# Middle stage of a long-convolution kernel: block stores issued by ScalarE, two steps after a block's last turn, instead of by the sync engine

## The reference

```python
h_mlp = np.maximum(pos_emb @ w1, 0.0) @ w2
h_filt = h_mlp * np.exp(-0.01 * pos)[:, None]
u = x * v
L = 2 * S
y = irfft(rfft(u, n=L, axis=1) * rfft(h_filt, n=L, axis=0)[None], n=L, axis=1)[:, :S, :]
t = (x * y).reshape(B * S, D)
h = t @ w_in                                    # 128 -> 2048
P = a[0] + a[1] * h + a[2] * h**2 + a[3] * h**3
Q = 1.0 + abs(b[0]) * abs(h) + abs(b[1]) * h**2
out = (P / (Q + 1e-6)) @ w_out                  # 2048 -> 128
```

## Time and profile before

| | |
|---|---|
| median of 3 runs | 2010.45 us (2007.9 to 2017.58) |
| the profiled execution, its time | 2015.76 us |
| its span, first to last instruction | 2014.0 us |
| mean granted TensorE clock, share of full | 0.99 |
| PE busy | 1909.8 us (95%) |
| DVE busy | 1735.1 us (86%) |
| ACT busy | 1643.8 us (82%) |
| POOL busy | 1737.2 us (86%) |
| queue q1 (SP), share of 16 DMA engines over the span | 28.0% |
| queue q10 (ScalarE), likewise | 4.7% |

### The profile page before, as it was taken

The page is one execution under the profiler, slowest core; times in us unless marked ns, Lnnn a source line. Parts: engine busy times, 40 slices in busy tenths (PEclk is TensorE's granted clock), DMA queues, the critical chain, the costliest instruction groups (busy, mean ns, idle before and its releaser), DMA issues. The chain is left out here.

```text
span 2014.0 us, 27071 instructions
## 1 busy us (share of the span) xinstructions
PE 1909.8 (95%) x7898; PEld 1301.4 (65%) x7898; DVE 1735.1 (86%) x2375; ACT 1643.8 (82%) x2424; POOL 1737.2 (86%) x1226
## 2 busy tenths in 40 slices
PE   6998799999799999999999999999999999999997
PEld 4555467777566666666666666666666666666664
DVE  4555479999599999999999999999999999999997
ACT  1222246555499999999999999999999999999998
POOL 5555367777499999999999999999999999999997
PEclk9999999999999999999999999999999999999999
DMA  7888889999601111111111111111111111111100
GB/s 195 276 289 290 248 204 248 248 255 247 183 5 33 33 34 34 38 46 38 38 33 33 34 33 34 33 34 33 34 33 34 33 34 33 34 33 37 34 9 13
DMA packets 77517, 181.83 MB, mean 90 GB/s; under 512 B 15565, under 2 KB 19557, under 8 KB 74485
## 3 DMA queue, kind: packets, MB, share of 16 engines
q1 hardware_dynamic: 70717, 144.74, 28.0%
q10 hardware_dynamic: 6656, 35.39, 4.7%
HBM read 108.36 MB, written 71.76 MB: 89 GB/s over the span
## 5 line engine op out<-in xcount | busy, mean ns | idle before, releaser
L726 POOL TENSOR_TENSOR den<-slope,mag 128x832 f32<-128x832 f32 x480 | 947.4, 1974 | 0.0
L962 PE MATMUL acc_p<-g_s,w_out_k 128*128 128x416 f32 x1920 | 768.8, 523 | 43.1 <-DVE g_s L879 22.6
L846 DVE SCALAR_TENSOR_TENSOR num<-square,level,h_p 128x832 f32<-128x832 f32 x480 | 517.8, 1079 | 83.9 <-ACT square L757 41.7
L718 POOL TENSOR_SCALAR slope<-mag,den_c 128x832 f32<-128x832 f32 x480 | 500.2, 1042 | 60.1 <-DVE mag L841 43.0
L962 PEld LDWEIGHTS acc_p<-g_s,w_out_k 128*128 128x128 f32 x1920 | 342.1, 189 | 290.2 <-issue 183.9
L879 DVE SCALAR_TENSOR_TENSOR g_s<-num,ratio,r_p 128x832 f32<-128x832 f32 x480 | 518.0, 1079 | 11.6 <-ACT r_p L773 4.6
L757 ACT ACTIVATE square<-h_p,centre 128x832 f32<-128x832 f32 x480 | 469.0, 977 | 39.3 <-DVE mag L841 36.7
L951 PE MATMUL h_p<-xy_hi,w_lo 128*128 128x416 f32 x960 | 454.3, 473 | 7.0 <-DVE num L846 5.6
L766 ACT ACTIVATE den<-den 128x832 f32<-128x832 f32 x480 | 440.9, 919 | 1.7 <-POOL den L726 1.5
L773 ACT ACTIVATE r_p<-den 128x832 f32<-128x832 f32 x480 | 426.8, 889 | 0.9 <-DVE g_s L879 0.7
L951 PE MATMUL h_p<-xy_hi,w_hi 128*128 128x416 f32 x960 | 336.9, 351 | 0.0
(11 more groups left out here) (79 smaller groups left out, 2190.4 us busy)
## 6 DMA issues: line engine op xcount, KB each, us to landing
bin_s<-bent SPq DMA_DIRECT2D x23, 1440.0 KB, 10.8
bent<-bent_s ACTq DMA_DIRECT2D x28, 1152.0 KB, 9.8
x_s<-in_x SPq DMA_DIRECT2D x59, 416.0 KB
vin_s<-back SPq DMA_DIRECT2D x29, 768.0 KB, 5.9
back<-back_s SPq DMA_DIRECT2D x23, 960.0 KB, 12.8
v_s<-in_v SPq DMA_DIRECT2D x30, 416.0 KB
out<-o_s SPq DMA_DIRECT2D x60, 208.0 KB
merged_s<-table_merged SPq DMA_DIRECT2D x24, 225.0 KB, 4.1
```

Of the source, the lines that this page charges most:

```text
L718: nc.gpsimd.tensor_scalar(slope[:, q % DEEP], mag[:, q % DEEP], den_c[:, 1:2], den_c[:, 0:1], ALU.mult, ALU.add).then_inc(slope_done, 1)
L726: nc.gpsimd.tensor_tensor(den[:, q % DEEP], slope[:, q % DEEP], mag[:, q % DEEP], ALU.mult).then_inc(den_done, 1)
L846: nc.vector.scalar_tensor_tensor(out=num[:, q % NUMS], in0=square[:, q % SQUARES], scalar=level[:], in1=h_p[:, q % 2, :, 0:TOK], op0=ALU.a ...
L962: mm = nc.tensor.matmul(acc_p[:, 0:TOK], w_out_k[:, ft], g_s[:, q % DEEP, t], start=(ft == 0), stop=(ft == FT - 1))
```

## The change

`store` of the middle stage is taken out of SP's stream and put into ScalarE's. ScalarE issues the store of block b in its iteration k = 4(b+1) + 1, behind cos_part(k), that is two steps after the block's last turn. What it waits for, what it writes and the semaphore it counts are the same. The four stores of the last block and the wait for all stores at the end stay with SP.

```diff
--- before.py
+++ after.py
@@ -452,12 +452,6 @@
                     sp.dma_start(bin_s[:, s].rearrange("p k c f -> p k (c f)"),
                                  bent[blk * JB:(blk + 1) * JB].rearrange("k j f -> j k f")).then_inc(bin_in[s], 16)
 
-                def store(blk):
-                    s = blk % SLOTS
-                    sp.wait_ge(vturned, (blk + 1) * JB)
-                    sp.dma_start(back[:, blk * JB:(blk + 1) * JB, :],
-                                 back_s[:, s].rearrange("p k c f -> p k (c f)")).then_inc(back_out[s], 16)
-
                 load_merged(0)
                 for m in range(JB):
                     sp.dma_start(bin_s[:, 0, m].rearrange("p c f -> p (c f)"), bent[m]).then_inc(first_in[m], 16)
@@ -476,7 +470,6 @@
                                          (unfold_s, tab["unfold"]), (w_in_s, w_in),
                                          (w_out_s, w_out.rearrange("(t p) d -> p t d", p=128))):
                             sp.dma_start(dst[:], src).then_inc(later_in, 16)
-                    store(blk)
                 for m in range(JB):
                     k = (K_BLOCKS - 1) * JB + m
                     sp.wait_ge(vturned, k + 1)
@@ -523,6 +516,12 @@
                     act.wait_ge(v_done, k + 1)
                     nc.scalar.activation(vpart[:, k % 2], v_p[0:J, k % 2], ACT.Copy,
                                          scale=turn_j[:, k, 0:1]).then_inc(vpart_done, 1)
+
+                def store(blk):
+                    s = blk % SLOTS
+                    act.wait_ge(vturned, (blk + 1) * JB)
+                    nc.scalar.dma_start(back[:, blk * JB:(blk + 1) * JB, :],
+                                 back_s[:, s].rearrange("p k c f -> p k (c f)")).then_inc(back_out[s], 16)
 
                 act.wait_ge(spread_in, SPREAD)
                 nc.scalar.activation(spread_hi[:], spread_s[:], ACT.Copy).then_inc(split_done, 1)
@@ -533,6 +532,8 @@
                         split_y(k + LEAD_Y)
                     if inside(k):
                         cos_part(k)
+                    if k >= JB + 1 and k % JB == 1:
+                        store(k // JB - 1)
                 act.wait_ge(later_in, LATER)
                 nc.scalar.activation(w_hi[:], w_in_s[:], ACT.Copy).then_inc(split_done, 1)
```

## The result

The changed kernel takes 2025.03 us (median of 7 runs, 2017.82 to 2028.51) against 2010.45 before (7 runs, 2005.77 to 2017.58): the ratio, estimated over all runs (that of the two medians is 1.0073), is 1.0068, 95% interval 1.0049 to 1.0087. Run again beside the experiments it was 1.0048 (1.0030 to 1.0066). So it is slower, by 0.5 to 0.7%, 10 to 14 us. The forecast was +4 us.

What follows compares the result with a forecast made beforehand. The middle stage was taken as bound by TensorE, with DMA just below its limit. From 2015.8 us profiled, +5 for loads, -1 for TensorE's waits and 0 otherwise gave +4, so 2014.5 against the 2010.45 median; range 2005 to 2028.

Steps and rivals of the forecast that it cites:

- the rival priced from +10 on: Middle stage slower by over 0.5%: two queues at once make DMA less efficient; +10 to +24 us, chance 0.22.
- part 3, the load of bin_s: Store packets delay the load's tail past its 11.61 us deadline: 0.25 us a block, 21 loads, +5 us.
- The picture of every block a little late: Expected sign: load landings about 12 us, short TensorE waits every fourth step, SP's issues 10.9 to 11.0 us apart.
- What bounds the kernel, and the worth of the hidden waits: Middle stage: TensorE sets 10.77 us a block; VectorE's 7.8 us of back_s waits are hidden, removing them gives about 1.2.
- Part 1, ScalarE's cost: ScalarE issuing 23 stores, 0.56 us each, behind cos_part and ahead of h_s; taken as 0, without cover 3 us.
- Part 2, the slot of back_s: Store issued later, 8.1 us left to its slot's deadline, lands in 5.7 to 7.1; VectorE's waits vanish, worth 1 us.
- 1.9 plus the mixed phase: Store's landing time: 1.9 us fixed plus the phase shared with a load, 5.7 to 7.1 us in all.
- the store misses the slot: Rival: from a landing 8.8 us after issue, each further us costs 22 us, 2032 at 9.8; chance 0.04.
- halving the excess: A wait at a block's first product also moves the next product fed, so half the load's +0.5 us stays: 0.25.
- Part 4, the end: Stage's ends: first loads precede any store, and store 22 lands at 525.5, before w_lo ends at 526.2; 0 us.
- the third rival: Slower by over 0.5%: mix moves only at 214 GB/s, load 2.3 us late, +24, 2034; chance 0.22.

Runs made afterwards that it cites:

- second execution: The changed kernel run and traced again with no edit; ratio to the kernel before 1.0048 (1.0030 to 1.0066).
- the kernel before with three slots of both: Kernel before the change, stores on SP, with three slots instead of two for bin_s, merged_s and back_s; ratio 0.9997 to before.
- one step of delay: Changed kernel, but ScalarE issues the store one step behind the block's last turn instead of two; ratio 1.0034 to the kernel before.
- three steps of delay: Changed kernel with three slots for back_s and ScalarE issuing the store three steps behind the block's last turn; ratio 1.0012 to the kernel before.

## Why the prediction was right, and where it was not

The direction held and the time lies in the stated range. The size was off: +4 forecast, +10 to +14 measured. That is the size of the rival priced from +10 on (chance 0.22), but not its mechanism, since the mix turned out not to be slower; and by the forecast's own line at 0.5% the outcome is "slower", which had 0.26, and not "same", which had 0.70. The step called decisive (part 3, the load of bin_s) stands behind five of the six long periods of the first execution. But a third slot for the store takes as much off the stretch (6 to 9 us) as one for the load (6 to 8), so that the slot of back_s, put at nothing, carries about half.

The picture of every block a little late did not come true. The store landed after 8.9 us and not after 6 or 7, VectorE's waits for back_s stayed, the median of the loads stayed at 10.8 us (11.4 in the second execution), TensorE waited for bin_s in five blocks of the steady part and not in each, and 14 of 20 periods stayed at 10.77 us. By its steps:

- **What bounds the kernel, and the worth of the hidden waits.** Right, by the kernel before with three slots of both.
- **Part 1, ScalarE's cost.** Taken as 0, and it is 0, but not for the reason given. The timeline of ScalarE, and the load before it on SP's:

```profile
324.50 0.63 ACT L513 ACTIVATE y_hi<-y_s 120x512 fp32r<-120x512 f32 x1 [1.10 <-PE v_p L589]
324.56 0.34 ACTq L523 DMA_DIRECT2D back<-back_s  x1
325.04 0.67 ACT L517 ACTIVATE vpart<-v_p,turn_j 120x512 f32<-120x512 f32 x1
325.71 0.39 ACT L506 ACTIVATE h_s<-x_p 120x256 f32<-120x256 f32 x1
...
320.69 0.82 SPq L452 DMA_DIRECT2D bin_s<-bent  x1
```

 The issue took 0.34 us, not 0.56, and ran while ScalarE was in y_hi: it comes before vpart, not behind it, and h_s at 325.71 still follows vpart (325.04 + 0.67) at once, as in the earlier trace rows. So the store was issued 4.2 us after T0 (320.32), not 5.4, and had 9.2 us to its deadline, not 8.1.

- **Part 2, the slot of back_s.** Wrong. The landing was put at 5.7 to 7.1 us; it was 8.9 in the mean, up to 11.2, and the waits did not vanish. The failed step is "1.9 plus the mixed phase": the store's packets were taken to start 0.6 us after its issue. In the DMA view of 324.9 to 328.9 us, with the store issued at 324.56, ScalarE's queue q10 moved one packet:

```profile
DMA packets 261, 0.81 MB, mean 202 GB/s; under 512 B 1, under 2 KB 1, under 8 KB 259
...
q1 hardware_dynamic: 259, 0.79, 96.0%
...
q10 hardware_dynamic: 1, 0.01, 0.8%
...
DMA packets 366, 1.07 MB, mean 227 GB/s; under 512 B 12, under 2 KB 40, under 8 KB 365
...
q1 hardware_dynamic: 365, 1.05, 98.3%
```

 Four us go by with almost only the load's packets. The last two lines are of the run with one step of delay, 368.8 to 373.5 us, with the store issued at 368.51: nothing on q10 for 4.7 us. The rival "the store misses the slot" had 0.04. With the earlier issue its bound moves from 8.8 to about 9.9 us (9.2 and the 0.7 that VectorE absorbs); three stores lay beyond it (10.6 and twice 11.2), and with a third slot the stretch was 6 to 9 us shorter. Its price of 22 us for each further microsecond is not tested, since only some blocks missed the slot.

- **Part 3, the load.** That a store beside the load delays it was right, three of the terms were not. The mixed phase runs faster than the fast end assumed, 393 GB/s (measured with one step of delay) against 354. But a load becomes late in some blocks only, so that the mean of all loads rises by just 0.6 us (11.1 to 11.7) while the late ones reach 14.8. And halving the excess, which holds where all loads are late alike (one step behind: 0.7 late in the median, half of it over 21 blocks is 7.3, measured 8.7), doesn't hold for loads that are late one at a time. The five loads that were late in the steady part (13.3, 13.0, 14.1, 12.2 and 13.4) exceed 11.61 by 8.0 us in all; the five periods in which they were awaited are 9.7 us too long together, 7.8 without the 1.9 of the next point. The whole excess is paid, not half.

- **A term that was missing: the clock.** The windows view after the longest wait of the steady part, and the matmul that ends it; then the matmul that ends the wait at the end of the stage, a window behind it, and a window of the second execution:

```profile
378.00:380.00 2.00, 0.47 (x2) 0.33 (x3) 0.37 (x1) 0.44 (x1) 1.94 (x2) 1.00 0.98 270
380.00:382.00 2.00, 2.00 (x10) 1.58 (x9) 1.34 (x3) 0.38 (x1) 0.00 (x0) 0.75 0.91 198
382.00:384.00 2.00, 2.00 (x9) 1.73 (x9) 1.31 (x4) 0.27 (x1) 0.73 (x1) 0.50 0.99 215
384.00:386.00 2.00, 2.00 (x11) 1.49 (x10) 1.03 (x3) 1.32 (x3) 1.28 (x1) 0.90 0.99 222
388.00:390.79 2.79, 2.79 (x19) 2.23 (x18) 2.56 (x6) 1.69 (x4) 1.67 (x2) 1.00 0.28 103
...
379.53 1.55 PE L603 MATMUL x_p<-bin_s,merged_s 120*120 120x384 f32 x4 [2.41 <-DMA bin_s<-bent]
...
494.79 2.92 PE L603 MATMUL x_p<-bin_s,merged_s 120*120 120x384 f32 x4 [3.03 <-DMA bin_s<-bent]
...
498.00:500.00 2.00, 2.00 (x11) 2.00 (x11) 1.78 (x4) 0.12 (x1) 0.40 (x1) 0.50 1.10 214
...
482.00:484.00 2.00, 2.00 (x7) 1.49 (x7) 0.78 (x3) 0.83 (x2) 0.85 (x2) 0.53 0.95 206
```

 After that wait the granted clock was 0.75 from 380 to 382 us and 0.50 from 382 to 384, that is 1.2 GHz, then 0.90. The period was 4.3 us too long, of which 2.4 are the wait; the other 1.9 go with the clock. At the end, after 3.0 us of waiting until 494.79, it was 0.50 from 494 to 500. The second execution has the same once (last line): after a wait of 2.2 us that ended at 478.99 the clock was 0.62 from 480 to 482 and 0.53 from 482 to 484, in its longest period, 14.87 us. The other long periods of the first execution, four of them with waits for bin_s too, had a clock of 1.00 in the mean. The forecast had costed waits at their own length.

- **Part 4, the end.** Wrong, 0 against +6.1 us in one execution and +1.9 in the other. It is no new mechanism: load 22, awaited behind the last T0, landed after 14.8 us and cost 3.0 us of waiting, and the six microseconds at half the clock behind it cost up to 3 more (an estimate from the clock of 0.50), which together is about the 6.1. Load 23 landed after 12.7 us, but nobody waited for it, and store 19 (11.2 us) held VectorE for 2.2 us at the same time. I had followed the last stores to their landing, but not the last loads, whose neighbours the stores also are.

That the range held is luck in part: its slow end, 2028, was taken from half of the third rival, in which the mix moves at 214 to 261 GB/s, and the mix ran at 393. It was wide enough for another reason than the one given.

**What stays open.** Why the store's packets don't start for 4 to 5 us: whether they queue behind the load where the transfers' descriptors are made, or in the DMA engines, no run tells. The time from the store's own issue is not what fixes it: with three steps of delay the store of 379.15 us, issued 6.6 us behind its load, had moved 2 packets (beside 135 of the load) by 381.4 and then went ahead, so that its packets start about 9 us behind the load's issue, as in the changed kernel. Nor is it known why some blocks are hit and others not. The row of landings looks as if each stall gives the next load an empty queue (DMA busy falls to 0.28 in the stretch up to 390.79) and a delay then builds up again over some blocks; that is argued, not shown.

The Trainium skill (DMA: Bandwidth & Descriptors, section "Rules for kernel authors") says of spreading DMAs over SP, ACT and GpSimd that it brings no bandwidth, since all run on the same 16 engines and interleave, and only saves issue time. The traces agree that nothing is gained, and add a price where both kinds have deadlines: 0.5 to 0.7% here. The forecast also weighed what the Trainium skill (same page, section "Queues, rings and completion order") says of turns, runs of about 9 to 17 descriptors from one queue before the next. The window with 90 packets beside 84 speaks against it, if a packet of the profile is a descriptor: 120 packets of a store over 16 engines are only about eight for one, at 0.31 us each 2.5 us in which the load would stand still, but the two queues went side by side at the window's start (15 and 14 packets from 375.0 to 375.5 us) and at its end (19 and 15 from 377.0 to 377.5).

## What to carry to other kernels

In one queue the transfer with the near deadline can be put first, and while one queue alone was in use no load here held TensorE for more than the 0.26 us of the kernel before; in two queues the packets mix, and the landing of the one that started first depends on what comes in beside it. Before moving an issue to another engine, compare for each transfer the latest landing (not the mean) with its deadline; with DMA engines over 0.9 busy and margins under 1 us, as here, keep one queue or pay for a slot more on both sides. Measure the stage by a stretch of the trace whose ends belong to it, since the span of the whole kernel moved by more, for other reasons, than the change did.

## What the hardware showed that was not expected

- In the blocks shown the transfer in the second queue moved almost nothing for 4 to 5 us after its issue while a large one of the first queue was under way (1 packet of 261; 2 us in the run with three steps of delay). With one step of delay packets of both queues then went one for one (90 and 84 in 2.5 us) at 393 GB/s, as fast as stores alone (402).
- A packet of the load takes half as long between packets of the store as among its own kind: in the mix 84 packets used 24.4% of the engines' time in 2.5 us, 0.12 us each, where the 423 of before, at 214 GB/s, used 97.3% of 6 us, 0.22 us each.
- An issue by ScalarE took 0.34 us and lay beside a running activation. It cost ScalarE nothing that the trace shows, with one store a block or with three transfers.
- TensorE's granted clock fell to 0.50 after waits of 2.4 and 3.0 us, for one window of 2 us and parts of its neighbours in the steady part and for 494 to 500 us at the end, and once in the second execution after a wait of 2.2 us (0.53 from 482 to 484 us).
